# Second MoE: its first product on pairs of token tiles, as seven block products and sums of blocks in place of eight block products

## The reference

```python
def _moe2_ref(x, w_in, w_out, g_ln) -> np.ndarray:   # x 2304x512, w_in 512x1024, w_out 1024x512
    h = x @ w_in
    h_max = np.max(h, axis=-1, keepdims=True)
    e = np.exp(h - h_max)
    sm = e / (np.sum(e, axis=-1, keepdims=True) + 1e-09)
    solu = h * sm
    mu = np.mean(solu, axis=-1, keepdims=True)
    var = np.mean((solu - mu) ** 2, axis=-1, keepdims=True)
    ln = (solu - mu) / np.sqrt(var + 1e-06) * g_ln
    return (ln @ w_out).astype(np.float32)
```

## Time and profile before

| | us |
|---|---|
| median of 3 runs | 999.86 (999.68 to 1000.23) |
| the profiled execution | 1000.2 |
| its span, first to last instruction | 998.4 |
| TensorE busy in the span | 976.0 |
| VectorE, ScalarE, GpSimd busy | 529.9, 415.6, 253.9 |
| last `up` of the first MoE ends, `hidden` of tile 0 starts | 768.9, 775.1 |

### The profile page before, as it was taken

The page is one execution under the profiler, slowest core; times in us unless marked ns, Lnnn a source line. Parts: engine busy times, 40 slices in busy tenths (PEclk is TensorE's granted clock), DMA queues, the critical chain, the costliest instruction groups (busy, mean ns, idle before and its releaser), DMA issues.

```text
span 998.4 us, 16512 instructions
## 1 busy us (share of the span) xinstructions
PE 976.0 (98%) x5844; PEld 925.7 (93%) x5844; DVE 529.9 (53%) x863; ACT 415.6 (42%) x739; POOL 253.9 (25%) x242
## 2 busy tenths in 40 slices
PE   5999999999999999999999999999999999999997
PEld 5999999999998999999999999999999778888886
DVE  6788788878778644322222222222223766556664
ACT  3777777777778543212112112112122422223221
POOL 2777787777878100000000000000000000000000
PEclk9999999999999999999999999999999999999999
DMA  6666666666761543110010010000021100000000
GB/s 176 160 159 162 156 160 160 158 158 157 173 143 53 168 130 96 32 33 1 0 32 0 0 32 0 0 0 0 0 84 43 41 22 21 21 24 28 21 22 32
DMA packets 51566, 71.31 MB, mean 71 GB/s; under 512 B 14552, under 2 KB 24920, under 8 KB 51536
## 3 DMA queue, kind: packets, MB, share of 16 engines
q1 hardware_dynamic: 51536, 70.94, 27.6%
HBM read 33.25 MB, written 5.32 MB: 39 GB/s over the span
## 4 chain that ended last, share of the span: by engine, by line
PE 92%; issue 3%; DVE 2%; DMA 1%; SPq 1%; ACT 1%; POOL 0%; POOLq 0%
PE PS L1114 12%; PE PS L1131 10%; PE PS L1132 10%; PE PS L1133 10%; PE PS L1076 9%; PE PS L1078 8%; PE PS L1199 5%; PE PS L1198 5%; PE PS L1200 5%; PE PS L1257 3%; PE PS L1259 3%; PE PS L1258 3%; PE PS L1233 3%; PE PS L1231 3%; PE PS L1232 3%
## 5 line engine op out<-in xcount | busy, mean ns | idle before, releaser
L532 POOL TENSOR_TENSOR p_lo<-prob,p_hi 128x576 fp32r<-128x576 f32 x144 | 207.9, 1445 | 50.8 <-ACT p_hi L612 48.9
L1076 PE MATMUL PS<-ops 128*128 128x288 f32 x642 | 182.2, 305 | 14.8 <-DVE ops L911 6.7
L1131 PE MATMUL PS<-x_hi,w_ab_rolled 128*128 128x384 f32 x576 | 192.5, 334 | 0.2 <-DVE w_ab_rolled L867 0.2
L1133 PE MATMUL PS<-x_hi,w_ab_rolled 128*128 128x384 f32 x576 | 192.4, 334 | 0.0
L1132 PE MATMUL PS<-x_lo,w_ab_rolled 128*128 128x384 f32 x576 | 192.4, 334 | 0.0
L1078 PE MATMUL PS<-ops 128*128 128x288 f32 x642 | 177.6, 298 | 0.0
L950 DVE TENSOR_TENSOR gate<-gate,PS 128x384 f32<-128x384 f32 x72 | 39.9, 554 | 251.9 <-ACT gate L716 251.9
L716 ACT ACTIVATE gate<-PS 128x384 f32<-128x384 f32 x72 | 35.4, 492 | 266.7 <-PE PS L1133 266.7
L1076 PEld LDWEIGHTS PS<-ops 128*128 128x128 f32 x642 | 122.6, 191 | 23.9 <-issue 12.3
L835 DVE TENSOR_REDUCE neg_max<-PS 128x1 f32<-128x576 f32 x144 | 108.5, 755 | 59.9 <-PE PS L1078 59.7
L1078 PEld LDWEIGHTS PS<-ops 128*128 128x128 f32 x642 | 122.8, 191 | 0.0
(11 more groups left out here) (91 smaller groups left out, 1523.6 us busy)
## 6 DMA issues: line engine op xcount, KB each, us to landing
qk_raw<-qkT_dram SPq DMA_DIRECT2D x32, 288.0 KB, 3.1
ops<-qk_hi SPq DMA_DIRECT2D x62, 144.0 KB
ops<-qk_hi SPq DMA_DIRECT2D x31, 288.0 KB
ops<-qk_lo SPq DMA_DIRECT2D x62, 144.0 KB
v_raw<-v_tiles_dram SPq DMA_DIRECT2D x32, 160.0 KB, 2.6
xT<-head_sb SPq DMA_DIRECT2D x32, 144.0 KB, 3.3
out_dram<-o_sb SPq DMA_DIRECT2D x18, 256.0 KB, 2.0
stage<-inverse_dram SPq DMA_DIRECT2D x20, 192.0 KB, 3.9
```

The source lines that it names most:

```text
L532: pool.tensor_tensor(p_lo[:, s, :], prob[:, s, :], p_hi[:, r, :].bitcast(F32), ALU.subtract).then_inc(p_lo_done, 1)
L1076: pe.matmul(ps[:, b, 0:HALF], weights[0][:, r, own], moving[0][:, r, cols], start=(n == 0), stop=False)
L1131: pe.matmul(bank, w[:, 0, :], x_hi[:, k, :], start=(k == 0), stop=False)
L1133: ins = pe.matmul(bank, w[:, 1, :], x_hi[:, k, :], start=False, stop=(k == NK - 1))
```

## The change

The first product of the second MoE now works on pairs of token tiles. Per pair p the operand is a block matrix A11, A12 (first tile, first and second half of the 512 inner rows), A21, A22 (second tile), and `w_in` is four blocks of 256 by 512. In place of eight block products of 6 matmuls each there are seven:

- A side: S1 = A21 + A22, S2 = S1 - A11, S3 = A11 - A21, S4 = A12 - S2. B side: T3 = B22 - B12, T2 = T3 + B11, T1 = B22 - T2 (which is B12 - B11), T4 = B21 - T2.
- Products: A11 B11, A12 B21, S2 T2, S3 T3, S1 T1, S4 B22, A22 T4, in this order, of 6 matmuls of 512 columns each. They go to the banks 1, 0, 3, 2, 3, 1, 2.
- Seven sums of 128x512 by VectorE (`add`) and one copy by ScalarE (`copy_first`) put them together in the banks 0 to 3 as the hidden values of both tiles.

Around it: the four sums of A blocks per pair (`sum_y`, 128x256 each) and the low parts of the seven A blocks (`low_y`: 512, 768, 256 and 256 columns) are GpSimd's, in place of VectorE's `low_y`; the high parts are three copies by ScalarE. The B sums (four of 128x1024) and the splitting of seven blocks in place of four are VectorE's and ScalarE's during the last chunk of the first MoE. `wout_raw` is asked for when the seven blocks are split. The last chunk of the first MoE is written out on TensorE behind a loop over the others. `hidden(0)`, for the pair 0, stands before `down` of the slices 10 and 11. In the loop over pairs TensorE does `hidden(p)`, with `turn` of the second tile of the pair before inside it, then `project` of both tiles of the pair before, then `turn` of the pair's first tile. There are two exponential buffers, `project` uses the banks 6 and 7 in turn, and the last tile is no longer turned and projected in two parts.

```diff
...
+        A11, A12, A22, S2, S3, S1, S4 = range(7)
         with ExitStack() as a:
-            y_hi = sb(a, "y_hi", [P, 2, NK, P], F32R)
-            y_lo = sb(a, "y_lo", [P, 2, NK, P], F32R)
-            h_negmax = sb(a, "h_negmax", [P, 1])
-            h_sum = sb(a, "h_sum", [P, 1])
+            ya_hi = sb(a, "ya_hi", [P, 7, 2, P], F32R)
+            ya_lo = sb(a, "ya_lo", [P, 7, 2, P], F32R)
...
+            win_sums = sb(a, "win_sums", [P, 3, 2, 2, BANK], F32R)
+            y_sums = sb(a, "y_sums", [P, 4, 2, P])
+            sum_a = sb(a, "sum_a", [P, BANK])
+            sum_b = sb(a, "sum_b", [P, BANK])
...
+        B11, B21, B22, T3, T2, T1, T4 = range(7)
+        def win(b):
+            return win_blocks[:, b] if b < 4 else win_sums[:, b - 4]
...
-            sp.wait_ge(ab_done, NCH * NF)
+            sp.wait_ge(win_lo, 7)
...
-            pool.wait_ge(y_done, NCH * NF)
+            def sum_y(p):
+                at_least(pool, ya_lo_done, 4 * p)
+                (a11, a12), (a21, a22) = ([y_block(p, i, slice(j, j + 1)) for j in range(2)] for i in range(2))
+                s2, s3, s1, s4 = (y_sums[:, n] for n in range(4))
+                pool.tensor_tensor(s1, a21, a22, ALU.add).then_inc(y_sum_done, 1)
+                pool.tensor_tensor(s3, a11, a21, ALU.subtract).then_inc(y_sum_done, 1)
+                pool.wait_ge(y_sum_done, 4 * p + 1)
+                pool.tensor_tensor(s2, s1, a11, ALU.subtract).then_inc(y_sum_done, 1)
+                pool.wait_ge(y_sum_done, 4 * p + 3)
+                pool.tensor_tensor(s4, a12, s2, ALU.subtract).then_inc(y_sum_done, 1)
+            def low_y(p, parts=range(4)):
+                for part in parts:
+                    if part == 0:
+                        pool.wait_ge(ya_hi_done, 3 * p + 1)
+                        pool.tensor_tensor(ya_lo[:, A11:A22].rearrange("p a k n -> p (a k) n"), y_block(p, 0, slice(0, 2)),
+                                           ya_hi[:, A11:A22].rearrange("p a k n -> p (a k) n").bitcast(F32),
+                                           ALU.subtract).then_inc(ya_lo_done, 1)
+                    elif part == 1:
+                        pool.wait_ge(ya_hi_done, 3 * p + 2)
+                        pool.tensor_tensor(ya_lo[:, S2:S4], y_sums[:, 0:3], ya_hi[:, S2:S4].bitcast(F32),
+                                           ALU.subtract).then_inc(ya_lo_done, 1)
+                    elif part == 2:
+                        pool.tensor_tensor(ya_lo[:, S4], y_sums[:, 3], ya_hi[:, S4].bitcast(F32),
+                                           ALU.subtract).then_inc(ya_lo_done, 1)
+                    else:
...
+            pool.wait_ge(ab_done, NF * (NCH - 1) + 10)
+            pool.wait_ge(y_out_act, (NK // 2) * 2)
+            pool.wait_ge(y_out_dve, (NK // 2) * 2)
+            sum_y(0)
+            pool.wait_ge(g_lo_done, NF * NCH)
+            pool.wait_ge(ab_done, NF * NCH)
+            low_y(0)
             pool.memset(halfpow[:, :], -0.5).then_inc(half_set, 1)
             pool.wait_ge(half_set, 1)
-            def rstd(i, j):
-                n = i * 2 + j
-                pool.wait_ge(var_done, n + 1)
-                pool.tensor_tensor(small[:, 3:4], small[:, 2:3], halfpow[:, :], ALU.pow).then_inc(rstd_done, 1)
-            with pool.Fori(0, NTT // 2) as i:
-                for j in range(2):
-                    rstd(i, j)
+            sum_y(1)
+            low_y(1, (0, 1))
+            rstd(0, 0)
+            low_y(1, (2, 3))
+            rstd(0, 1)
+            pool.wait_ge(y_out_act, (NK // 2) * (NCH + 1))
+            pool.wait_ge(y_out_dve, (NK // 2) * (NCH - 1))
+            sum_y(2)
+            for p in range(1, TOK // (2 * P)):
+                rstd(p, 0)
+                if p + 1 < TOK // (2 * P):
+                    low_y(p + 1)
+                rstd(p, 1)
+                if p + 2 < TOK // (2 * P):
+                    sum_y(p + 2)
...
+            def copy_first(p):
+                act.wait_ge(h_part, 7 * p + 1)
+                at_least(act, h_summed, 7 * p - 2)
+                act.activation(sum_a[:, :], PS[:, 1, :], ACT.Copy).then_inc(h_copied, 1)
...
+            def pair_tiles(p, final=False):
+                copy_first(p)
+                high_normed(p - 1, 1)
+                expo_step(p, 0)
+                expo_step(p, 1)
+                if not final:
+                    high_y(p + 1)
+                out_copy(p - 1, 0)
+                if final:
+                    high_normed(p, 0)
+                out_copy(p - 1, 1)
+                if not final:
+                    high_normed(p, 0)
...
+            high_y(0)
+            copy_first(0)
+            expo_step(0, 0)
+            high_y(1, (0,))
+            expo_step(0, 1)
+            high_y(1, (1, 2))
+            y_out(NCH - 1, range(NK))
+            copy_first(1)
+            high_normed(0, 0)
+            high_wout()
+            high_normed(0, 1)
+            expo_step(1, 0)
+            expo_step(1, 1)
+            high_y(2)
+            out_copy(0, 0)
+            out_copy(0, 1)
+            high_normed(1, 0)
...
+                if f == 6:
+                    low_win(B11)
+                    low_win(B21)
+                if f == 7:
+                    low_win(B22)
+                    sum_win(T3, B22, T3, ALU.subtract)
+                if f == 8:
+                    sum_win(T2, T3, B11, ALU.add)
+                    low_win(T3)
+                if f == 9:
+                    sum_win(T1, B22, T2, ALU.subtract)
+                    sum_win(T4, B21, T2, ALU.subtract)
+                if f == 10:
+                    low_win(T2)
+                    low_win(T1)
+                if f == 11:
+                    low_win(T4)
...
+            def add(p, step, part, out, bank, other):
+                dve.wait_ge(h_part, 7 * p + part)
+                if step > 0:
+                    dve.wait_ge(h_summed, 7 * p + step)
+                dve.tensor_tensor(out, PS[:, bank, :], other[:, :], ALU.add).then_inc(h_summed, 1)
+            def early_sums(p, steps=range(3)):
+                for step in steps:
+                    if step == 0:
+                        dve.wait_ge(h_copied, p + 1)
+                        add(p, 0, 2, PS[:, 0, :], 0, sum_a)
+                    elif step == 1:
+                        add(p, 1, 3, sum_a[:, :], 3, sum_a)
+                    else:
+                        add(p, 2, 4, sum_b[:, :], 2, sum_a)
+            def late_sums(p):
+                add(p, 3, 5, sum_a[:, :], 3, sum_a)
+                add(p, 4, 5, PS[:, 3, :], 3, sum_b)
+            def hidden_sums(p):
+                add(p, 5, 6, PS[:, 1, :], 1, sum_a)
+                hidden_max(p, 0)
+                add(p, 6, 7, PS[:, 2, :], 2, sum_b)
+                hidden_max(p, 1)
...
+            def tiles(p):
+                hidden_sums(p)
+                solu_step(p, 0)
+                norm_step(p, 0)
+                normed_step(p, 0)
+                dve.wait_ge(normed_done, 2 * p + 1)
+                solu_step(p, 1)
+                if isinstance(p, int) and p == 0:
+                    early_sums(1, (0,))
+                    stats_step(p, 1)
+                    early_sums(1, (1,))
+                    small_steps(p, 1)
+                    early_sums(1, (2,))
+                else:
+                    norm_step(p, 1)
+            def pair_tiles(p):
+                low_normed(p - 1, 0)
+                early_sums(p)
+                late_sums(p)
+                low_normed(p - 1, 1)
+                tiles(p)
+                normed_step(p, 1)
+            early_sums(0)
+            late_sums(0)
+            tiles(0)
+            normed_step(0, 1)
+            low_normed(0, 0)
+            late_sums(1)
+            low_wout(range(NK2))
+            low_normed(0, 1)
+            tiles(1)
+            normed_step(1, 1)
+            last = TOK // (2 * P) - 1
+            with dve.Fori(2, last) as p:
+                pair_tiles(p)
+            pair_tiles(last)
+            low_normed(last, 0)
+            low_normed(last, 1)
...
+            def product_of(p, a, b, bank, first=False):
+                if first:
+                    pe.wait_ge(win_lo, b + 1)
+                for k in range(2):
+                    high, low = ya_hi[:, a, k, :], ya_lo[:, a, k, :]
+                    pe.matmul(PS[:, bank, :], high, win(b)[:, 0, k, :], start=(k == 0), stop=False)
+                    pe.matmul(PS[:, bank, :], high, win(b)[:, 1, k, :], start=False, stop=False)
+                    ins = pe.matmul(PS[:, bank, :], low, win(b)[:, 0, k, :], start=False, stop=(k == 1))
+                ins.then_inc(h_part, 1)
+            def hidden(p, turns=(), first=False):
+                pe.wait_ge(ya_lo_done, 4 * p + 1)
+                at_least(pe, solu_done, 2 * p - 1)
+                product_of(p, A11, B11, 1, first)
+                product_of(p, A12, B21, 0, first)
+                if len(turns) == 2:
+                    pe.wait_ge(y_out_act, (NK // 2) * (NCH + 1))
```

(89 more changed lines are left out.)

291 lines of the change are left out of this document (121 added, 170 removed).

## The result

The changed kernel takes 1001.8 us, median of 20 runs (998.82 to 1003.67), against 1000.24 (999.08 to 1002.34, 20 runs) for the kernel before; the ratio is 1.0014, interval 1.0008 to 1.0020. The 54 matmuls that it saves bring nothing: it is slower by about 0.14%, 0.8 to 2.0 us. The profiled execution took 1002.5 us, its span is 1000.7.

A forecast was written before the change was run, and what follows sets the result against it. TensorE's matmuls bound the second MoE: span 998.4 - 12.6 saved + 15.5 new waits + 0.5 restarts - 4.2 old waits = 997.6, plus 1.46 to the median, about 999.0 us; own range 997 to 1001, wide range 995.5 to 1005.5.

The forecast's parts named there:

- The bound: Second MoE: TensorE's matmuls bound it, so matmuls taken out shorten it if the other engines come in time.
- The saving: `hidden` of a pair: 42 matmuls in place of 48, 1.40 us less per pair, 12.6 us for nine.
- the faster rival: Overlap costs less (1.9 us) or products run at `project`'s pace (1.7 us): each 997.2, both 995.4; chance 0.33.
- VectorE's sums: Loop: seven 128x512 sums out of PSUM, 0.72 us each when waiting for the one ahead, 5.0 us per pair.
- normed: VectorE, twice per pair: 0.81 us plus 0.55 for GpSimd's work beside it, bounds 0 and 1.1 us more.
- The second rival: VectorE bounds the loop once `normed` costs over about 0.75 us more: 1001.6 to 1007 us; chance 0.20.
- GpSimd: Per pair four sums and low parts of 4.6 us; in time no bound, but its work lies beside VectorE's.
- The waits: TensorE at both ends of the second MoE: 15.5 us in ten waits, the longest 3.3, 2.1, 3.9 and 3.45.
- The clock: 0.09: Rival: TensorE's clock falls in a gap of over 3 us, 1.7 us or twice that: 1001 to 1003; chance 0.09.

The follow-up runs named there:

- fill_all: The changed kernel with extra 512-column matmuls on TensorE in the four gaps where it waits; 996.78 us, ratio 0.9972 to the kernel before.
- The forced gaps: The kernel before, TensorE held up in seven loop rounds by 3 or 6 short GpSimd additions; 1010.05 us with three, 1024.68 us with six.
- orders: The changed kernel with only the order of work round the four gaps changed, no extra matmuls; 995.82 us, ratio 0.9959 to the kernel before.
- orders_fill: The changed kernel with the order of work round the four gaps changed, plus extra matmuls in what is left of the gaps; 995.88 us.

## Why the prediction was wrong, step by step

The time lies within 0.2% of the kernel before and within the wide range of 995.5 to 1005.5, but above the forecast's own range, 997 to 1001, and on the slower side, where I forecast 0.9 us faster. The working named the right bound and the right waits. It failed in its sum, which has no term for the clock.

- *The bound.* TensorE, by its matmuls: right. The kernel before with 54 fewer gained 11.1 us.
- *The saving.* 1.40 us per pair was too little. The pair takes 22.19, against 22.46: 24 matmuls of `hidden` took 5.55 us and 18 took 4.17, 0.2268 apart behind a first one that costs 0.1 more, against 5.66 for 24 before. So the half of the faster rival that spoke of `project`'s pace came true, about 2.3 us over nine pairs.
- *VectorE's sums.* 0.72 forecast, 0.69 measured, into PSUM and into SBUF alike: the upper bound of 0.06 more wasn't needed.
- *`normed`.* 0.55 more each, 0.33 on the mean: about 0.66 for the first of a pair, 0.16 for the second. The second rival, VectorE as the bound from 0.75 on, didn't come; no wait in the loop. The Trainium skill, in GPSIMD Engine Reference, section Key points, names VectorE's instructions that use both ports or have two SBUF inputs. The traces agree: `normed` 0.81 alone and 1.14 on the mean beside GpSimd, and `wout_lo_sb`, with two SBUF inputs, 0.74 to 2.31 beside GpSimd, the sums out of PSUM 0.69 throughout.
- *GpSimd.* 512 columns 1.28 forecast and 1.30 measured (2.16 for pair 0's, beside VectorE, where I had added 0.5); 768 columns 1.90 and 2.29. In the loop it fitted.
- *The waits.* 3.3, 2.1, 3.9 and 3.45 forecast; 3.6, 1.6, 3.8 and 3.5 measured, 12.5 in all, with the releasers that I named, the first one by its times only. The short ones were 0.8 in place of 2.7.
- *The step that failed: the clock.* The sum 998.4 - 12.6 + 15.5 + 0.5 - 4.2 puts it at nothing, and the chances say "The clock: 0.09". What the runs show in its place is 7.4 us of slow matmuls, of which 5.8 reach the span (`fill_all`). In the profiled execution it fell in four of four gaps, and I had weighed it by the absence of a fall in the trace of before, where the longest wait is 1.4 us. The forced gaps show that this absence said nothing: of the same kernel's gaps those of 1.3 us left the clock up seven times in seven, and those of 2.1 brought it down six times in seven. My price, 1.7 us per fall, was near the 1.56 measured, though it doesn't follow from its own count: 16 matmuls at 0.2 us more are 3.2. The rows show eight or nine. The Trainium skill, in TensorE: Matmul & The Clock Gate, section The HAM clock gate, says that an idle TensorE goes back to half clock; the trace agrees (granted clock 0.50, distance 0.43 us), and it should have weighed more than rows of a trace that held no such gap.

Put together: my span of 997.6, less 2.2 for the shorter waits, less 2.3 for the pace, plus 7.4 for four falls is 1000.5, and 1000.7 was recorded. Two errors in the good direction hid most of the one in the bad: that the forecast came within 0.3% is luck. (One more slip, on which nothing hangs: the wide range ends at 1005.5 for VectorE at 1.1, where the rival's own sum gives 1004.4.) Without the falls the change would have been faster by about 0.3%, as the filled kernel is.

Open are why the products of `hidden` now start 0.2268 us apart, and what decides whether the clock falls behind a wait. In the second MoE of the profiled executions of all these kernels, idle times of TensorE of 3.2 to 4.1 us let it fall nine times in ten, those of 2.3 three times in four, the forced ones of 1.88 six times in seven. Of those from 1.2 to 1.7 us only two did: the 1.65 of the changed kernel, which left the clock up in four of its variants, and the 1.27 of `orders`, which left it up in `orders_fill`.

## What to carry to other kernels

When TensorE is the bound, a wait that replaces matmuls isn't an even exchange: from about 2 us on, and at times below, the clock can fall behind it. Price each such gap with that, here 1.5 to 2.7 us, even if the trace of before shows no fall. Close such gaps by order (a product or half a `project` that is ready anyway) before counting what a saving of matmuls brings; where nothing is ready, idle matmuls into a free bank are a cheap way to see what the clock costs. When work is moved to fill a gap, look at which instruction of the neighbour engine it will then lie beside.

## What I had not expected of the hardware

- Matmuls whose result nobody reads made the kernel 5.0 us faster, 996.78 against 1001.8.
- After one gap the slow stretch begins at once (`turn` 1.62 us in place of 0.80), after another 1.2 us later; the slow rows take 3.65, 3.64, 5.6 and 3.0 us behind the four gaps.
- A 512-column VectorE instruction with two SBUF inputs took up to 2.31 us beside one 768-column instruction of GpSimd, against 0.74 alone.
